# Attention, routed experts and a feed-forward in one launch: the turn tables move from VectorE to GpSimd, and the rank products go one chunk later

## Chip, cores and metric

One core of a Trainium2 chip runs the whole program in one launch. The metric is the device time in microseconds, the median of several runs. The profiled execution is one more, with its own time. Engines are named as in the profile: PE (TensorE), DVE (VectorE), ACT (ScalarE), POOL (GpSimd), SP (SyncE, which only issues DMAs here).

## What is computed

A linear attention with a decaying state over 768 steps (batch 4, 8 heads of 48), its rows as 3072 tokens of 384 into a top-1 mixture of 8 experts, and a dense feed-forward with an ELU:

```python
for t in range(S):
    kt, vt, rt = (k[:, :, t], v[:, :, t], r[:, :, t])
    cur = np.einsum('bhd,bhe->bhde', u[None] * kt, vt)
    y[:, :, t] = np.einsum('bhd,bhde->bhe', rt, state + cur)
    state = w[None, :, :, None] * state + np.einsum('bhd,bhe->bhde', kt, vt)
...
expert_idx = np.argmax(x @ w_gate, axis=1)
for e in range(E):
    mask = expert_idx == e
    out[mask] = gate_w[mask, None] * (np.maximum(x[mask] @ w1[e], 0.0) @ w2[e])
...
g = np.where(h > 0.0, h, np.exp(np.minimum(h, 0.0)) - 1.0)   # h = x @ w_in
return g @ w_out
```

## The kernel before

Every engine has its own program, written out by hand; within one the order is that of the code, and between them only semaphores order the work. There are three stages.

**Attention** (to about 156 us). The 768 steps are cut into 6 chunks of 128, for 4 batches b: 24 chunks n = 6b + c. Per chunk PE makes the scores (`heads`, line 1348), the state products (`new_state`, line 1369, which need `v_in`), what the old state gives (`old`, 1382, which needs `xT` of the chunk before), the rows and gate logits of the chunk before (`rows_logits`, 1407), the own term (`own_sum`, 1359) and the masked part (`inside`, 1393). DVE scales the next chunk's r and k, masks the scores, renews the state, reduces the logits (`lgt`), and makes `own` and `xT`. POOL scales the keys (`keys`, tile `kn_s`), makes `rk` and scatters finished rows, tagged with token and gate, into `x_sorted` in HBM, expert by expert. SP loads r, k, kn, vT and v of the chunks to come into pairs of buffers: in its round n `load_rk(n + 1)`, which waits for `scaled` and `rk_done`, then `load_v(n)`, then a piece of expert weights.

Once per batch, at c = 0, DVE chooses experts (`choose`, which ends with the one-hot `hot`), PE turns `hot` into ranks within each expert (`ranks`, lines 1421 to 1424, into PSUM), and DVE makes row numbers and gates of them (`place`, from `rank_e` to the reciprocal). The last batch is placed in two groups, the first four chunks at c = LAST = 4, the other two after the end.

While the attention runs, the weights of two experts are loaded in 24 pieces and split into a high and a low part (`expert_highs` on ACT, `first_experts` on POOL). Pieces 0 to 11 are of expert 0. Pieces 12 to 23 are of the fullest other expert after two batches: DVE's `pick_first` finds it at chunk FIRST = 12, from the counts that `ranks` leaves in PSUM, and signals `first_ok`; SP waits for that in its round 14 and reads the expert into a register. In which order the experts take their turns, and where their tiles begin, follows in five steps on DVE, `turns_a` to `turns_e`, in chunks 13 to 17. `split_now` says which pieces are split in chunk n: before chunk 12 piece n, from 14 on piece n - 2, and pieces 22 and 23 after the last chunk.

**Expert tiles** (156 to 462 us). 31 tiles of 128 rows. Per tile: gather `xg` (ACT issues it), transpose (`x_pose`, line 1457), split into hi and lo, up product (`first_up` or `up`), relu, transpose `hs` (`h_pose`, 1487), split into `hThi` (ACT) and `hTlo` (DVE), down product. Tile 0 is of the picked expert and needs no table. For the others DVE computes tables from the final counts: `fill_row` (where each expert's rows end), `past`, `tile_row`, `tile_turn`, `end_i`, `tile_start`. SP fills the rows behind each expert's last with zeros, eight DMAs in the order of turns: two as soon as `fill_row` is there (`fill_in`), the others when all scatters have landed (`fill2_in`, and `fills_in` for the last five), and then loads the weights of turn 2. ACT may gather tile i only when the fills that it could touch are in; for i = 3 it waits for all of them.

**Feed-forward** (462 to 880 us), with which the change has nothing to do.

## Time and profile before

| | us |
|---|---|
| runs | 893.85, 893.48, 890.81 (median 893.48) |
| the profiled execution | 888.82 |
| its span, first to last instruction | 887.1 |
| PE busy in it | 851.8 (96%) |
| DVE, ACT, POOL busy | 411.5, 246.4, 399.2 |
| mean granted TensorE clock | 0.992 |

The span is that of one execution, 1.7 us shorter than its time. Busy times overlap; an engine that is idle may be waiting or have nothing to do. In the timeline a row is a start, a duration, an engine, a line of the kernel and what it writes and reads; a bracket at its end is how long the engine sat idle before it and what released it. SPq and ACTq are the DMA issues of an engine, whose durations are those of the issue, not of the transfer. DVE was busy for 11.2 of the 12 us from 82 to 94.

### The profile page before, as it was taken

The numbers are of one execution on the slowest core, as the hardware profiler recorded it, in microseconds if no ns is written. First come the engines' busy times: TensorE is split into PE (matmuls) and PEld (weight loads), VectorE is DVE, ScalarE is ACT, GpSimd is POOL, SyncE is SP. The second block draws the span as 40 slices with busy tenths as digits, with TensorE's granted clock in tenths as the row PEclk, the third lists the DMA queues.
The fourth block names the chain that finished last, engine by engine and source line by source line (L and its number), as shares of the span: only waits on it lengthen the run. The fifth ranks groups of instructions, "written<-read, shape, count | busy, mean of one in ns | idle before, by whom it ended". The sixth has DMA issues, their size and how long they took to land.

```text
span 887.1 us, 16841 instructions
## 1 busy us (share of the span) xinstructions
PE 851.8 (96%) x5278; PEld 770.8 (87%) x5278; DVE 411.5 (46%) x842; ACT 246.4 (28%) x514; POOL 399.2 (45%) x286
## 2 busy tenths in 40 slices
PE   5999989879999999999999999999999999999996
PEld 5888988669999999999988899988999989998895
DVE  7888997625444444434335553332333232332221
ACT  3333232212222222222223343222332223232221
POOL 7677677207575734437102223423423422433424
PEclk9999999989999999999999999999999999999998
DMA  7877986353445335164121000100100100000000
GB/s 181 235 230 235 238 237 192 126 178 117 149 145 177 118 117 176 48 228 147 37 63 45 19 19 10 45 19 1 54 18 1 44 27 0 35 0 0 36 1 36
DMA packets 48991, 83.96 MB, mean 95 GB/s; under 512 B 6816, under 2 KB 27040, under 8 KB 48544
## 3 DMA queue, kind: packets, MB, share of 16 engines
q1 hardware_dynamic: 35808, 60.59, 22.8%
q10 hardware_dynamic: 10048, 13.04, 4.6%
q0 software_dynamic: 3072, 9.46, 2.8%
q8 instruction: 42, 0.69, 0.3%
q14 instruction: 21, 0.17, 0.1%
HBM read 65.92 MB, written 17.15 MB: 94 GB/s over the span
## 4 chain that ended last, share of the span: by engine, by line
PE 78%; issue 12%; DVE 4%; POOL 3%; DMA 2%; SPq 1%; POOLq 0%; ACT 0%; ACTq 0%; DVEq 0%
PE bank L1462 10%; PE bank L1464 10%; PE bank L1463 9%; PE bank L1574 6%; PE bank L1576 6%; PE bank L1575 6%; PE bank L1593 5%; PE bank L1595 5%; PE bank L1594 5%; PE bank L1487 3%; PE bank L1393 2%; PE bank L1348 2%; PE bank L1382 2%; PE bank L1407 2%; POOL glo L669 2%
## 5 line engine op out<-in xcount | busy, mean ns | idle before, releaser
L669 POOL TENSOR_TENSOR glo<-gf,ghi 128x512 fp32r<-128x512 f32 x96 | 123.8, 1290 | 303.9 <-ACT ghi L1291 303.9
L1072 DVE TENSOR_SCALAR he<-he 128x512 f32<-128x512 f32 x96 | 41.0, 427 | 241.0 <-ACT he L1309 240.9
L1309 ACT ACTIVATE he<-bank 128x512 f32<-128x512 f32 x96 | 57.5, 599 | 253.5 <-PE bank L1576 253.5
L1593 PE MATMUL bank<-wout_hi,ghi 128*128 128x384 f32 x376 | 126.1, 335 | 0.3 <-issue 0.3
L1595 PE MATMUL bank<-wout_hi,glo 128*128 128x384 f32 x376 | 126.1, 335 | 0.0
L1594 PE MATMUL bank<-wout_lo,ghi 128*128 128x384 f32 x376 | 126.0, 335 | 0.0
L1574 PE MATMUL bank<-x2hi,win_hi 128*128 128x512 f32 x288 | 115.7, 402 | 0.0
L1576 PE MATMUL bank<-x2hi,win_lo 128*128 128x512 f32 x288 | 114.1, 396 | 0.0
L1575 PE MATMUL bank<-x2lo,win_hi 128*128 128x512 f32 x288 | 113.5, 394 | 0.0
L1462 PE MATMUL bank<-w_sb,hThi 128*128 x248 | 87.5, 353 | 4.8 <-DVE hTlo L938 2.9
L1464 PE MATMUL bank<-w_sb,hTlo 128*128 x248 | 84.6, 341 | 0.0
L1463 PE MATMUL bank<-w_sb,hThi 128*128 x248 | 84.6, 341 | 0.0
L1593 PEld LDWEIGHTS bank<-wout_hi,ghi 128*128 128x128 f32 x376 | 70.7, 188 | 4.7 <-issue 0.7
L1594 PEld LDWEIGHTS bank<-wout_lo,ghi 128*128 128x128 f32 x376 | 70.6, 188 | 4.5
L1462 PE MATMUL bank<-w_sb,xhi 128*128 x180 | 73.1, 406 | 1.0 <-issue 1.0
L1595 PEld LDWEIGHTS bank<-wout_hi,glo 128*128 128x128 f32 x376 | 70.6, 188 | 0.0
L1464 PE MATMUL bank<-w_sb,xlo 128*128 x180 | 70.6, 392 | 0.0
L1463 PE MATMUL bank<-w_sb,xhi 128*128 x180 | 70.1, 389 | 0.0
L1076 DVE SCALAR_TENSOR_TENSOR gf<-bank,he 128x512 f32<-128x512 f32 x96 | 66.4, 692 | 3.7
L1576 PEld LDWEIGHTS bank<-x2hi,win_lo 128*128 128x128 f32 x288 | 54.1, 188 | 13.3
L1219 ACT ACTIVATE hThi<-bank 128x512 fp32r<-128x512 f32 x62 | 33.7, 596 | 104.3 <-PE bank L1487 104.3
L1574 PEld LDWEIGHTS bank<-x2hi,win_hi 128*128 128x128 f32 x288 | 54.2, 188 | 9.1 <-issue 0.4
(214 smaller groups left out, 1502.5 us busy)
## 6 DMA issues: line engine op xcount, KB each, us to landing
w_raw_up<-w SPq DMA_DIRECT2D x12, 768.0 KB, 6.2
w_raw_down<-w SPq DMA_DIRECT2D x12, 768.0 KB, 7.0
w_raw<-w SPq DMA_DIRECT2D x24, 256.0 KB, 4.1
y_rows<-ye ACTq DMA_DIRECT2D x31, 192.5 KB, 2.5
xg<-x_sorted ACTq DMA_DIRECT2D x30, 193.0 KB, 2.8
k_in<-kT SPq DMA_DIRECT2D x48, 96.0 KB, 3.4
r_in<-rT SPq DMA_DIRECT2D x48, 96.0 KB, 3.7
kn_in<-kn SPq DMA_DIRECT2D x24, 192.0 KB, 3.8
```

The source lines that it names most:

```text
L669: pool.tensor_tensor(glo[f % GS][:, :], gf[f % 2][:, :], ghi[f % GS][:, :].bitcast(F32), ALU.subtract).then_inc(s.g_lo, 1)
L1076: dve.scalar_tensor_tensor(gf[f % 2][:, :], bank[1 + f % 2][:, :], 0.0, he[f % 2][:, :], ALU.max, ALU.add).then_inc(s.g_done, 1)
L1309: act.activation(he[f % 2][:, :], bank[1 + f % 2][:, :], ACT.Exp).then_inc(s.exp_done, 1)
L1462: pe.matmul(out, hi, w, start=first, stop=False)
L1463: pe.matmul(out, hi, w_low, start=False, stop=False)
L1464: return pe.matmul(out, lo, w, start=False, stop=last)
L1574: pe.matmul(bank[1 + f % 2][:, :], win_hi[:, k, cols], x2hi[par][:, k, :], start=(k == 0), stop=False)
L1575: pe.matmul(bank[1 + f % 2][:, :], win_hi[:, k, cols], x2lo[par][:, k, :], start=False, stop=False)
L1576: last = pe.matmul(bank[1 + f % 2][:, :], win_lo[:, k, cols], x2hi[par][:, k, :], start=False, stop=(k == KD - 1))
L1593: pe.matmul(to, ghi[f % GS][:, rows], wout_hi[:, f, :], start=(f == 0), stop=False)
L1594: pe.matmul(to, ghi[f % GS][:, rows], wout_lo[:, f, :], start=False, stop=False)
L1595: last = pe.matmul(to, glo[f % GS][:, rows], wout_hi[:, f, :], start=False, stop=(f == KF2 - 1))
```

## The change

It touches the order of the work in the attention, who makes the turn tables, and the passage to the expert tiles.

1. `ranks` and `place` move from chunk c = 0 to c = 1 (and from LAST to LAST + 1): PE multiplies behind the next chunk's scores, DVE places between that chunk's `own` and `xT`. `pick_first` moves from chunk 12 to 13. SP's wait for `first_ok` stays in round 14.
2. `turns_a` to `turns_e` are taken off DVE. POOL makes the same tables in one go in round 15 (`turn_tables`, 29 instructions, six waits on its own semaphore), after its split and before its scatter, plus two helper values, `row_step` and `other_row`.
3. Splits run one chunk closer: pieces 12 and 13 in chunk 14, then n - 1, and 22 and 23 in chunk 23, on ACT, POOL and in SP's rounds (where the order of the loads stays as it was).
4. SP reads all eight turns into registers ahead of the fills; the fourth fill signals `fill3_in` on its own.
5. DVE makes `next_row`, the row of tile 1, early from the first expert's count (four instructions more), and puts `gid` and `hTlo` of tile 0 ahead of `past`. ACT gathers tile 1 by `next_row`, and gathers tile 3 before the relu of tile 1.

```diff
         def split_now(n):
-            return [n] if n < FIRST else ([n - 2] if n >= FIRST + 2 else [])
+            if n < FIRST:
+                return [n]
+            if n < FIRST + 2:
+                return []
+            return {FIRST + 2: [n - 2, n - 1], NT - 1: [n - 1, n]}.get(n, [n - 1])
@@ SP @@
+            sp.wait_ge(s.turns_ok, 1)
+            turns = [sp.value_load(turn_expert[0:1, turn:turn + 1], min_val=0, max_val=E - 1) for turn in range(E)]
             def fill(turn, done):
-                e = sp.value_load(turn_expert[0:1, turn:turn + 1], min_val=0, max_val=E - 1)
+                e = turns[turn]
...
             fill(2, s.fill2_in)
-            for turn in range(3, E):
+            fill(3, s.fill3_in)
+            for turn in range(4, E):
                 fill(turn, s.fills_in)
@@ POOL, batch @@
+                    if n == FIRST + 3:
+                        turn_tables()
...
+            def turn_tables():
+                pool.wait_ge(s.first_ok, 1)
+                pool.tensor_scalar(pull[:, :], most[:, :], float(P), None, ALU.is_lt)
+                pool.tensor_scalar(is_first[:, :], iota_e[:, :], first[:, 0:1], None, ALU.is_equal)
...
+                pool.tensor_tensor(ahead[:, :, :], turn_of[:, :].unsqueeze(1).to_broadcast([P, E, E]),
+                                   turn_of[:, :].unsqueeze(2).to_broadcast([P, E, E]), ALU.subtract)
...
+                pool.tensor_copy(turn_expert[:, :], self_1[:, :])
+                pool.tensor_tensor(row_step[:, :], row_step[:, :], first_mul[:, :], ALU.add).then_inc(s.turns_ok, 1)
@@ DVE, batch @@
-                    if c == 0 and not fresh:
+                    if c == 1 and not fresh:
                         place(0, NC, b - 1, b - 1, b > 2)
-                    if last and c == LAST:
+                    if last and c == LAST + 1:
                         place(0, LAST, b, b, True)
                     x_columns(n, c % 2, fresh and c < 2)
-                    if n == FIRST:
+                    if n == FIRST + 1:
                         pick_first()
-                    if FIRST < n <= FIRST + 5:
-                        (turns_a, turns_b, turns_c, turns_d, turns_e)[n - FIRST - 1]()
@@ DVE, routing @@
+            rlink(dve.tensor_tensor(from_first[:, :], n_e[:, :], is_first[:, :], ALU.mult))
+            rlink(dve.tensor_reduce(n_first[:, :], from_first[:, :], AX.X, ALU.add))
+            rlink(dve.tensor_scalar(n_first[:, :], n_first[:, :], float(P), row_step[:, 0:1], ALU.is_gt, ALU.mult))
+            dve.tensor_scalar(next_row[:, :], n_first[:, :], other_row[:, 0:1], None, ALU.add).then_inc(s.next_row_ok, 1)
...
+            gate_and_id(0, 0, True)
+            v_hT(0, 0, True)
             rlink(dve.tensor_tensor(past[:, :, :], index[:, :].unsqueeze(2).to_broadcast([P, NI, E]),
...
-            gate_and_id(0, 0, True)
-            v_hT(0, 0, True)
@@ ACT @@
+            act.wait_ge(s.next_row_ok, 1)
+            act.wait_ge(s.fill_in, 32)
+            load_x(1, 1, next_row)
             act.wait_ge(s.rows_ok, 1)
-            act.wait_ge(s.fill_in, 32)
-            load_x(1, 1)
             act.wait_ge(s.fill2_in, 16)
             next_x(2, 0)
             a_x(1, xhi[1], True)
+            act.wait_ge(s.fill3_in, 16)
+            next_x(3, 1)
             a_relu(1, 1, True)
             a_x(2, xhi[0], False)
             a_hT(1, 1, True)
-            act.wait_ge(s.fills_in, 16 * (E - 3))
-            next_x(3, 1)
@@ PE, batch @@
+                    if c == 1 and b:
+                        ranks(NC, b - 1)
+                    if last and c == LAST + 1:
+                        ranks(LAST, b)
                     if c < NC - 1:
                         new_state(b, c, c % 2)
                     old(b, c, c % 2).then_inc(s.old_done, 1)
                     rows_logits(n - 1, (c - 1) % 2, fresh and c == 1)
                     own_sum(n, c % 2, False)
-                    if c == 0:
-                        ranks(NC, b - 1)
-                    if last and c == LAST:
-                        ranks(LAST, b)
```

On PE, in chunk 12, before: from `own_sum` (`rk`) to the scores of chunk 13; `hot` is the one-hot, `allb` and `ltri` are constant matrices.

```order
L1359 MATMUL bank<-rk_97,spread_u 128x128 x4
L1421 MATMUL bank<-hot_116,allb 128x8 x7
L1422 MATMUL bank<-hot_116,ltri 128x48
L1424 MATMUL bank<-hot_116,allb 128x48
L1424 MATMUL bank<-hot_116,allb 128x40
L1424 MATMUL bank<-hot_116,allb 128x32
L1424 MATMUL bank<-hot_116,allb 128x24
L1424 MATMUL bank<-hot_116,allb 128x16
L1424 MATMUL bank<-hot_116,allb 128x8
L1393 MATMUL bank<-am_101,v_in_91 48x128 x8
L1348 MATMUL bank<-r_s_94,k_s_96 128x128 x8
```

The same place after; the scores of chunk 13 are the row with `r_s_95`, and line numbers are those of the changed kernel:

```order
L1381 MATMUL bank<-rk_98,spread_u 128x128 x4
L1415 MATMUL bank<-am_102,v_in_92 48x128 x8
L1370 MATMUL bank<-r_s_95,k_s_97 128x128 x8
L1443 MATMUL bank<-hot_117,allb 128x8 x7
L1444 MATMUL bank<-hot_117,ltri 128x48
L1446 MATMUL bank<-hot_117,allb 128x48
L1446 MATMUL bank<-hot_117,allb 128x40
L1446 MATMUL bank<-hot_117,allb 128x32
L1446 MATMUL bank<-hot_117,allb 128x24
L1446 MATMUL bank<-hot_117,allb 128x16
L1446 MATMUL bank<-hot_117,allb 128x8
L1391 MATMUL bank<-v_in_93,kn_s_101 112x96 x4
```

The products stood ahead of `inside` (`am`) of chunk 12; now `inside` and the next scores go first and the products stand between these and the state products.

On DVE, from `own` of chunk 12 on, before:

```order
L750 TENSOR_TENSOR own_103<-vT_in_87,bank 128x512
L808 TENSOR_TENSOR rank_e<-bank,hot_116 128x48
L810 TENSOR_REDUCE rank<-rank_e 128x6
L816 SCALAR_TENSOR_TENSOR pos_i_58<-bank,rank 128x6
L818 TENSOR_REDUCE l_sum<-l_exp 128x6
L820 RECIPROCAL xt<-l_sum 128x6
L770 TENSOR_TENSOR xT_105<-bank,own_103 128x512
L832 TENSOR_REDUCE most<-bank 128x1
L833 SCALAR_TENSOR_TENSOR from_first<-bank,most,rev_in 128x7
L834 TENSOR_REDUCE rev_best<-from_first 128x1
L835 TENSOR_SCALAR first<-rev_best 128x1
L836 CAST first_expert<-first 128x1
```

After, `own` and `xT` of chunk 12 follow each other, and this stands in chunk 13, from its `own` on:

```order
L805 TENSOR_TENSOR own_105<-vT_in_89,bank 128x512
L863 TENSOR_TENSOR rank_e<-bank,hot_117 128x48
L865 TENSOR_REDUCE rank<-rank_e 128x6
L871 SCALAR_TENSOR_TENSOR pos_i_58<-bank,rank 128x6
L873 TENSOR_REDUCE l_sum<-l_exp 128x6
L875 RECIPROCAL xt<-l_sum 128x6
L825 TENSOR_TENSOR xT_107<-bank,own_105 128x512
L887 TENSOR_REDUCE most<-bank 128x1
L888 SCALAR_TENSOR_TENSOR from_first<-bank,most,rev_in 128x7
L889 TENSOR_REDUCE rev_best<-from_first 128x1
L890 TENSOR_SCALAR first<-rev_best 128x1
L891 CAST first_expert<-first 128x1
```

`place` (`rank_e` to `xt<-l_sum`) and `pick_first` (`most` to `first_expert`) are one whole chunk of DVE's work further back; what stood behind them, the scaling of the next chunk, now runs ahead of them.

On ACT, around the relu of tile 1 (`hs`), before; `xg_182` is the gather of tile 2, `xg_183` that of tile 3:

```order
L1199 DMA xg_182<-x_sorted 128x386
L1145 ACTIVATE xhi_127<-bank 128x384
L1212 ACTIVATE hs_131<-bank 128x512
L1145 ACTIVATE xhi_126<-bank 128x384
L1219 ACTIVATE hThi_133<-bank 128x512 x2
L1198 TENSOR_LOAD tile_row
L1198 ISA x2
L1199 ISA
L1199 DMA xg_183<-x_sorted 128x386
```

After, with `xg_189` for tile 2 and `xg_190` for tile 3:

```order
L1219 DMA xg_189<-x_sorted 128x386
L1167 ACTIVATE xhi_128<-bank 128x384
L1218 TENSOR_LOAD tile_row
L1218 ISA x2
L1219 ISA
L1219 DMA xg_190<-x_sorted 128x386
L1232 ACTIVATE hs_132<-bank 128x512
L1167 ACTIVATE xhi_127<-bank 128x384
L1239 ACTIVATE hThi_134<-bank 128x512 x2
```

The gather of tile 3 stood behind the relu, the split of tile 2 and `hThi` of tile 1; now it stands directly behind the split of tile 1's rows (`xhi`).

## Rows read from the trace of the kernel before

**Rows 1.** The page, part 1: busy us (share of the span) and instructions of each engine.
```profile
PE 851.8 (96%) x5278; PEld 770.8 (87%) x5278; DVE 411.5 (46%) x842; ACT 246.4 (28%) x514; POOL 399.2 (45%) x286
```

**Rows 2.** Timeline, PE: start us, us, engine line op out<-in xcount; chunks 13 and 15.
```profile
88.01 1.16 PE L1348 MATMUL bank<-r_s,k_s 48*128 48x128 f32 x16
...
100.63 1.02 PE L1369 MATMUL bank<-v_in,kn_s 128*112 128x96 f32 x8
```

**Rows 3.** Timeline, PE: rank products of chunks 6, 12, 18; in brackets the wait before.
```profile
51.79 0.18 PE L1422 MATMUL bank<-hot,ltri 128*128 128x48 bf16 x1 [0.86 <-DVE hot L798]
...
86.58 0.32 PE L1421 MATMUL bank<-hot,allb 128*128 128x8 bf16 x7 [0.67 <-DVE hot L798]
...
123.80 0.18 PE L1422 MATMUL bank<-hot,ltri 128*128 128x48 bf16 x1 [1.27 <-DVE hot L798]
```

**Rows 4.** Timeline, PE: waits for VectorE in chunks 15 and 17.
```profile
104.81 1.08 PE L1393 MATMUL bank<-am,v_in 128*48 128x128 f32 x16 [0.45 <-DVE am L743]
...
113.06 1.13 PE L1382 MATMUL bank<-r_s,state 128*128 128x128 f32 x8 [0.29 <-DVE xT L770]
...
116.70 1.08 PE L1393 MATMUL bank<-am,v_in 128*48 128x128 f32 x16 [0.72 <-DVE am L743]
```

**Rows 5.** Timeline, DVE and SyncE's queue: the chosen expert, and v of chunk 15.
```profile
89.57 0.15 DVE L836 CAST first_expert<-first 128x1 int32<-128x1 f32 x1
...
95.02 0.35 SPq L431 DMA_DIRECT2D v_in<-vn  x1
```

**Rows 6.** DMA issues of 95.0 to 95.3 us: KB each, us from issue to landing.
```profile
v_in<-vn SPq DMA_DIRECT2D x1, 192.0 KB, 4.4
```

**Rows 7.** Instructions of tile v_in: its DMAs' landing times.
```profile
DMA to landing us min/median/max: 2.4/3.7/5.2
```

**Rows 8.** Timeline, DVE: place of chunk 12, and own of chunk 13.
```profile
87.23 0.20 DVE L808 TENSOR_TENSOR rank_e<-bank,hot 128x48 f32<-128x48 f32 x1
...
88.13 0.69 DVE L770 TENSOR_TENSOR xT<-bank,own 128x512 f32<-128x512 f32 x1
...
93.08 0.69 DVE L750 TENSOR_TENSOR own<-vT_in,bank 128x512 f32<-128x512 f32 x1
```

**Rows 9.** Timeline, POOL and DVE: small and large instructions.
```profile
43.48 0.14 POOL L544 IOTA iota_e<- 128x8 f32 x1
...
100.76 1.28 POOL L583 TENSOR_TENSOR w_sb<-w_raw,w_sb 128x512 fp32r<-128x512 f32 x1
...
100.94 1.19 DVE L849 TENSOR_TENSOR ahead<-turn_of 128x64 f32<-128x64 f32 x1
...
203.58 6.82 POOL L576 TENSOR_TENSOR w_sb<-w_raw_up,w_sb 128x3072 fp32r<-128x3072 f32 x1 [0.19 <-POOL w_sb L573]
```

**Rows 10.** Instructions of tile kn_in: ns min/median/max, first and last start.
```profile
L564 POOL TENSOR_TENSOR kn_s<-kn_in,pw_kn x24: 991/1001/1020, 13.2 to 142.0; 128x384 f32<-128x384 f32 x24
```

**Rows 11.** Timeline, DVE and SyncE's queue, after the attention.
```profile
159.70 0.95 DVE L972 TENSOR_TENSOR fill_row<-n_e,first_row 128x8 int32<-128x8 f32 x1
...
162.13 14.12 SPq L463 DMA_DIRECT2D x_sorted<-zeros  x8
```

**Rows 12.** Timeline, PE: the first product of first_down.
```profile
166.06 0.68 PE L1462 MATMUL bank<-w_sb,hThi 128*128 x1 [2.88 <-DVE hTlo L938]
```

**Rows 13.** Windows: us, busy us by engine, PEclk (1.00 is 2.4 GHz), DMA share, GB/s.
```profile
166.00:168.00 2.00, 1.95 (x6) 1.95 (x7) 1.72 (x8) 0.00 (x0) 0.00 (x0) 0.50 0.28 97
...
189.00:191.00 2.00, 2.00 (x6) 2.00 (x7) 0.37 (x1) 0.00 (x0) 0.00 (x0) 0.50 0.31 112
```

**Rows 14.** Timeline, PE: x_pose of i=3, then x_pose and down around i=4.
```profile
187.35 0.90 PE L1457 MATMUL bank<-ident,xg 128*128 128x128 f32 x3 [3.54 <-DMA xg<-x_sorted]
...
200.13 0.49 PE L1457 MATMUL bank<-ident,xg 128*128 128x128 f32 x3
...
200.37 0.42 PE L1462 MATMUL bank<-w_sb,hThi 128*128 x1
```

**Rows 15.** The chain that ended last: start us, us, what.
```profile
179.56 7.75 DMA xg<-x_sorted
```

83 lines of the change are left out of this document (45 added, 38 removed).

## Prediction

> **What bounds the kernel now.** I read the page first: PE is busy for 96% of the span [rows 1], so a change of other engines' work pays only where PE waits. Then I looked for PE's waits in the timeline. From 195 us to the end the trace shows PE almost without one (the loop over sorted tiles has none), so the change can act only in the attention chunks (23 to 156 us) and in the passage to the expert tiles (156 to 193 us). In the attention two undisturbed chunks and one set of scores take 12.62 us (88.01 to 100.63) [rows 2], that is 5.76 a chunk. PE waits there for two reasons: at the rank products of chunks 6, 12 and 18 (and 22), for `hot` (0.86, 0.67, 1.27) [rows 3], and behind the turn steps that VectorE (DVE) fits into chunks 13 to 17 (0.45 in chunk 15, 0.29 and 0.72 in chunk 17) [rows 4]. In the passage it waits 2.88 us for `hTlo` and 3.54 us for the gathered tile `xg` of i=3, and after both gaps the granted clock is half, 1.2 GHz [rows 12 to 14].
>
> **Part 1, ranks one chunk later.** Behind the scores of the next chunk, `hot` is long there: in chunk 12 the products began at 86.58, the scores of 13 stand at 88.01 and last 1.1. The products themselves (0.25 to 0.42 us) stay. Gain 0.86+0.67+1.27 = 2.8 us. The wait of chunk 22 is given back: `place` for it now stands in chunk 23 between `own` and `xT`, and the last logits wait for that `xT`; `place` takes 1.3 us there, about what the waits around it took. Zero.
> `place` in the other batches is 0.90 us from `rank_e` to `xT` (87.23 to 88.13) [rows 8]. In chunks 7 and 13 it fits: `xT` then starts 6.8 to 7.0 us after the chunk's scores, and the next chunk's state product needs it at 8.0. In chunk 19, where it waits for slots (1.6 us in the profile), `xT` is 0.3 us late. Cost 0.3.
>
> **Part 2, turn steps off DVE.** Gain 0.45+0.29+0.72 = 1.5 us in chunks 15 and 17.
>
> **Part 3, the new lateness of `first_expert`.** SyncE's queue (SP) waits for `first_ok` in its round 14, and that wait is not moved, but `pick_first` is, from chunk 12 to chunk 13, behind that chunk's `own`, the `place` and `xT`. Queued behind the wait are the weight pieces 12 and 13, then k, r, kn of chunk 16, and v of chunk 15. Let T be the start of chunk 13's scores (88.01). Now: `first_expert` is done at 89.72, T+1.71; v of chunk 15 goes out at 95.02, 5.30 us after it, without a pause between its DMAs, and lands 4.4 us later at 99.4 [rows 5, 6]; PE needs it at 100.63 [rows 2]. Slack 1.2 us. Then: `own` of chunk 13 starts at T+5.07 (93.08) [rows 8] plus 0.42 for the rank products that now precede it, T+5.49; 0.59 to `place`, 0.90 to `xT`, and 1.59 from the start of `xT` to the end of `first_expert` (88.13 to 89.72): T+8.57. v goes out at T+13.87 and lands at T+18.27. PE is ready for it at 12.62 + 0.42 = T+13.04. **PE waits 5.2 us.** The bounds: landing in 3.7 us (median of v) 4.5; with 5.2 (longest) 6.0 [rows 7]. After gaps of 2.9 and 3.5 us the clock was half for 3 to 4 us of work [rows 13]; in the second the first twelve products took 4.0 us, where twelve at full clock take 2.1. So 1.8 us more. Cost 7.0 us, none of it in the trace of before. ScalarE and GpSimd (POOL) wait for the late pieces 12 and 13 too, but until T+14.9 and T+16.3 only, under PE's wait.
>
> **Part 4, turn tables on POOL.** 29 small instructions and six waits for its own results, in round 15, ahead of a scatter and of keys and `rk` of chunk 17, on which SP's loads for chunk 19 wait, and behind those v of chunk 18. The trace has no such instruction. From below: IOTA on 128x8 takes 0.14, the seven of them one every 0.1 us [rows 9], giving 3.5 us with the waits (0.19 each, as between POOL's own splits (203.58) [rows 9]). From above: two points of its elementwise form, 1.0 us for 384 columns and 1.28 for 512 [rows 9, 10], leave some 0.2 at nothing, giving 7.5. I take 5.3, between them, since pipelined starts are nearer to the IOTA row. Starting at T+21.6 (piece 14 lands at T+19.5, its split ends then), `rk` of chunk 17 is done 3.4 us after the tables, T+30.3, v of chunk 18 goes out 3.3 us later and lands at T+37.5; PE wants it at T+36.5. Cost 1.0 (0 to 3.2); no cost up to 4.3 us of tables. In chunk 19 POOL must wait for the later `place` before its two scatters, which sets v of chunk 22 back: 0.6 (0 to 0.9).
> A row on how the two engines meet: DVE's `ahead`, 64 columns, took 1.19 us and ended at 102.13, where POOL's subtraction ended at 102.04 [rows 9]; `fill_row` took 0.95 [rows 11] with POOL's last splits running until 160.63. The Trainium skill ("SBUF — State Buffer", section "Who interferes with whom") has it that a VectorE instruction with two SBUF inputs waits for a GpSimd instruction that reads SBUF, and that whichever came first holds the shared port. By that rule `fill_row` shrinks to 0.2, since those splits are now earlier; if the 0.95 were its own, the gain of part 5 would be 0.5 us less. The big VectorE instructions of a chunk read PSUM, so by the rule they don't hold the tables up.
>
> **Part 5, the passage.** (a) `hTlo` of tile 0 stands behind the tile tables; now ahead of `past`. `hThi` is ready at 163.3 and 163.9, four added instructions (0.9 us) take the place of the 0.75 that `fill_row` loses, so the two `hTlo` (0.64 each) end at 164.65 rather than 165.79: first_down starts 1.15 us earlier. PE's gap becomes 1.75 us (from 163.17). The clock fell within gaps of 2.9 and 3.5 us and not in one of 1.27 [rows 3, 12 to 14]; I take that it stays up, 1.4 us more. (b) `xg` of i=3 is issued at 179.56, after 3 MB of weights from 177.04 on, and lands 7.75 us later; PE is ready at 183.66 and begins at 187.35 [rows 14, 15]. Now it is issued ahead of relu(1), when `gid` of tile 1 and the fourth fill are there, at about 171, and has 10 us. Its wait goes, and with it the half clock: the twelve products after it ended at 192.98; at the pace of i=4 (200.13, 200.37) [rows 14] (0.24 and 12 x 0.175 us) they end at 186.0. Gain 7.0. (c) Fills go from 1.8 us apart (eight in 14.12) [rows 11] to some 1.1, one register load less. The second fill then lands at about 164.1, the last scatter at 164.4, `xg` of i=1 goes out at 165.1 and lands 2.7 later at 167.8; the earlier first_down reaches its transposition after 18 products, at 168.0. Just in time. It also starts the weights at 171.3; POOL needs these at 200 only. Nothing by itself. What is late next: PE itself. Sum 1.15+1.4+7.0 = 9.5 us.
>
> **Sum**, against the profiled execution (888.82 us, span 887.1): -2.8 -1.5 +7.0 +0.3 +1.0 +0.6 -9.5 = -4.9 us, 883.9. The median of the runs shown is 4.66 above that execution; the same 0.55% off 893.48 gives **888.6**.
>
> **Rivals.**
> *The loads come in time.* SP has been still for 8 us, so transfers could land faster, in 2.4 us as the fastest v did, with POOL light: waits of 3 us without the clock falling long, or less. Or the wait is hidden in a way I don't see. Without part 3: -4.9 -7.0 = -11.9 us, 881.6. For it: DMA was busy all along before this burst and is idle now. Against: the issue times alone (T+13.87) are past PE's T+13.03.
> *POOL and SP don't catch up.* Tables at 7.5 us, the v of chunk 18 3 us late and the clock falling again, first_down's clock gain missing: -4.9 +2.2 +1.8 +1.4 = +0.5, 894. For it: POOL then has splits, tables and scatters in a row, and the loads wait for `rk`.
> *Slower.* POOL's tables alone, if its small instructions take 0.45 us each: 13 us of tables put the v of chunk 18 out by 9 us, and a second half-clock stretch: -4.9 +8 +1.8 = +4.9, 898.4. It decides from 13 us of tables on. Against: the IOTA of 8 columns takes 0.14 [rows 9].
> *It doesn't do what it says.* `xg` of i=3 could still be late, if the fourth fill or `gid` of tile 1 came after the weights and it landed no sooner; it would need 11 us against the 7.75 seen. Then -4.9 +7 = +2.1, 895.6. I give it 3 of 100.
>
> **How the numbers follow.** The forecast as worked (-2.5 to -7.5) 50%; in time 20%; not catching up 20%; slower 5%; doesn't do what it says 3%; else 2%. A measurement tells about 0.5%, 4.5 us, from no change; the forecast lies just beyond, so I count 35 of its 50 as faster and 15 as same. Faster 0.35+0.20+0.02, same 0.15+0.17+0.02, slower the rest. Range: from the case without the wait, 881, to the one without catching up, 894, with 2 in 10 left out.
>
> **What would show it.** PE's `v_in` product of chunk 15 with a DMA wait of 4 to 6 us and half clock after it, SP's `v_in` issue some 14 us after chunk 13's scores; no wait at the rank products; tables on POOL in 4 to 7 us; `hTlo` of tile 0 ahead of `past`, PE's gap 1.8 us at full clock; no wait for `xg` at i=3. I am wrong if chunk 15 runs through, if the tables take over 10 us, or if something after 195 us moves.

## The result, and the profile after

The changed kernel took 897.96 us (median of 12 runs, 895.65 to 902.39), the kernel before 891.38 us on the same chip (12 runs, 888.98 to 893.85): **ratio 1.0079, 95% interval 1.006 to 1.0097**, slower by some 7 us where 4.9 less were forecast. The forecast's range ended at 894. The profiled execution took 900.95 us with a span of 899.2; a second profile of the same kernel (a0 below) is of an execution of 893.28 us with a span of 891.6. The median of 897.96 lies between the two, so both are read below.

The page of after, part 1; [rows 1] answer to it. PE has 4.3 us more busy time for the same number of instructions, at a mean granted clock of 0.985 against 0.992:

```profile
span 899.2 us, 16856 instructions
PE 856.1 (95%) x5278; PEld 775.5 (86%) x5278; DVE 407.5 (45%) x827; ACT 247.6 (28%) x514; POOL 405.0 (45%) x315
```

The timeline of after, PE, where it waits in the attention, and the rank products of chunk 13. Columns as in the rows of before:

```profile
83.26 1.71 PE L1391 MATMUL bank<-v_in,kn_s 128*112 128x96 f32 x8 [1.87 <-DMA v_in<-vn]
90.85 0.18 PE L1444 MATMUL bank<-hot,ltri 128*128 128x48 bf16 x1
107.62 1.81 PE L1391 MATMUL bank<-v_in,kn_s 128*112 128x96 f32 x8 [4.97 <-DMA v_in<-vn]
130.87 1.81 PE L1391 MATMUL bank<-v_in,kn_s 128*112 128x96 f32 x8 [4.88 <-DMA v_in<-vn]
158.09 1.47 PE L1391 MATMUL bank<-v_in,kn_s 128*112 128x96 f32 x8 [1.85 <-DMA v_in<-vn]
```

The rank products wait for nothing now (against 0.67 to 1.27 us in [rows 3]). In their place PE waits for v in chunks 12, 15, 18 and 22 (and 0.65 us in chunk 10). The windows of after at chunk 15 show the clock behind such a wait (the number after POOL's):

```profile
core 0: us, PE busy (x) PEld busy (x) DVE busy (x) ACT busy (x) POOL busy (x), PEclk, DMA share, GB/s
107.60:109.60 2.00, 1.98 (x10) 1.99 (x11) 0.75 (x2) 0.63 (x1) 1.69 (x3) 0.50 1.08 234
109.60:111.60 2.00, 2.00 (x15) 2.00 (x15) 0.52 (x2) 0.00 (x0) 2.00 (x4) 0.72 1.05 312
111.60:113.60 2.00, 2.00 (x27) 1.84 (x26) 1.07 (x3) 1.45 (x5) 1.77 (x8) 1.00 1.05 290
```

A chunk lasts from its scores to the next chunk's. Worked out from the starts of the scores in both timelines:

| chunk | before, us | after, us | more |
|---|---|---|---|
| 12 | 81.08 to 88.01 | 80.23 to 89.56 | 2.40 |
| 15 | 99.54 to 105.83 | 101.48 to 113.74 | 5.97 |
| 18 | 117.71 to 125.06 | 124.83 to 137.31 | 5.13 |
| 22 | 142.35 to 148.97 | 155.08 to 164.38 | 2.68 |
| start of first_up | 156.67 | 172.81 | 16.14 |

The four chunks make 16.18 us, as much as the whole attention lost; what the other chunks gained (the rank products of chunk 6, the turn steps of chunk 17) and lost (chunk 10) cancels. The passage gives some of it back.

Why v was late is in POOL's and SP's queues. POOL in after, three places: the first scatter of a batch, in POOL's round 13, the turn tables (first and last of 29 instructions), and what follows them; then SP's loads behind `rk`:

```profile
97.44 1.01 POOL L610 DMA_INDIRECT x_sorted<-xt,pos_i  x1 [7.36 <-issue]
...
110.78 0.25 POOL L647 TENSOR_SCALAR pull<-most 128x1 f32<-128x1 f32 x1
...
117.84 0.19 POOL L676 TENSOR_TENSOR row_step<-row_step,first_mul 128x1 f32<-128x1 f32 x1
118.76 1.11 POOL L610 DMA_INDIRECT x_sorted<-xt,pos_i  x1 [0.73 <-PE bank L1381]
119.90 1.01 POOL L577 TENSOR_TENSOR kn_s<-kn_in,pw_kn 128x384 f32<-128x384 f32 x1
120.86 1.28 POOL L571 TENSOR_TENSOR rk<-r_in,k_in 128x512 f32<-128x512 f32 x1
```

```profile
122.17 0.33 SPq L427 DMA_DIRECT2D k_in<-kT  x1
...
125.41 0.39 SPq L445 DMA_DIRECT2D v_in<-vn  x1
```

POOL stands 7.36 us at the scatter (1.86 in the kernel before, its row at 89.22), until `place`, now one chunk further back in DVE's order, is done (its last instruction ends at 96.42). The same scatter stands 5.04 us in round 7 and 6.14 in round 19. The keys and `rk` of the chunks to come are queued behind it, SP waits for `rk` with its next load of k, and v is queued behind that. The tables take 7.25 us; k goes out as soon as `rk` ends (122.14), v 3.24 us later, and it lands 5.4 us after that (the prediction had counted 3.9), when PE has stood 4.88 us.

The passage in after: relu of tile 0 on ACT, then PE at first_down, at up of tile 2 and at the gathered tile i=3, for which it doesn't wait:

```profile
180.60 0.60 ACT L1248 ACTIVATE hs<-bank 128x512 f32<-128x512 f32 x1 [7.07 <-remote]
```

```profile
184.19 0.68 PE L1484 MATMUL bank<-w_sb,hThi 128*128 x1 [1.79 <-DVE hTlo L956]
198.48 0.50 PE L1484 MATMUL bank<-w_sb,xhi 128*128 x1 [0.77 <-issue]
202.72 0.49 PE L1479 MATMUL bank<-ident,xg 128*128 128x128 f32 x3
```

The gap before first_down is 1.79 us (2.88 in [rows 12]). From the start of `up` of tile 2 to the end of the span it takes 899.2 - 198.48 = 700.7 us, where before took 887.1 - 179.45 = 707.65: 6.9 us less, since x of tile 3 is there. ACT began the relu at 180.60, though the last product of first_up ended at 177.48: 3.1 us that nothing in the trace accounts for.

### The profile page after: what moved, and what is told of

The parts are those of the page before. It is cut to its first block, busy times and chain, and to the rows that moved or that the text cites. A ratio compares the mean times of both kernels' runs of the same rounds, so it can differ in the third digit from the quotient of the medians.

```text
span 899.2 us, 16856 instructions
## 1 busy us (share of the span) xinstructions
PE 856.1 (95%) x5278; PEld 775.5 (86%) x5278; DVE 407.5 (45%) x827; ACT 247.6 (28%) x514; POOL 405.0 (45%) x315
## 4 chain that ended last, share of the span: by engine, by line
PE 75%; issue 12%; POOL 5%; DMA 4%; SPq 2%; DVE 1%; another core or an unknown queue 1%; ACT 0%; POOLq 0%; DVEq 0%; ACTq 0%
PE bank L1484 10%; PE bank L1486 9%; PE bank L1485 9%; PE bank L1596 5%; PE bank L1597 5%; PE bank L1598 5%; PE bank L1615 5%; PE bank L1616 5%; PE bank L1617 5%; PE bank L1509 3%; DMA v_in<-vn 3%; PE bank L1404 2%; POOL glo L724 2%; PE bank L1391 2%; PE bank L1429 2%
## 5 line engine op out<-in xcount | busy, mean ns | idle before, releaser
L1598 PEld LDWEIGHTS bank<-x2hi,win_lo 128*128 128x128 f32 x288 | 54.1, 188 | 13.1
```

Of the source, the lines that this page charges most:

```text
L1598: last = pe.matmul(bank[1 + f % 2][:, :], win_lo[:, k, cols], x2hi[par][:, k, :], start=False, stop=(k == KD - 1))
```

## Experiments

Each part alone, from the kernel before; then parts mended, from the kernel after. Ratios are to the kernel before on the same chip, and 0.001 is 0.9 us.

| kernel | ratio | 95% interval |
|---|---|---|
| the change | 1.0079 | 1.006 to 1.0097 |
| a0, the change again | 1.009 | 1.0058 to 1.0121 |
| p1, ranks alone | 1.0137 | 1.0101 to 1.0173 |
| p2, passage alone | 0.9935 | 0.9911 to 0.9959 |
| p3, tables alone | 1.0029 | 1.0014 to 1.0045 |
| p4, splits alone | 0.9985 | 0.9972 to 0.9998 |
| x1, pieces later | 1.0026 | 1.0009 to 1.0043 |
| x2, scatters later | 1.0028 | 1.0011 to 1.0044 |
| x3, tables in pieces | 1.001 | 0.9992 to 1.0027 |
| x4, all three | 0.9932 | 0.9907 to 0.9957 |
| x5, x4 and v first | 0.9915 | 0.9882 to 0.9948 |
| x8, x1 + x2, tables on DVE | 0.9979 | 0.996 to 0.9999 |
| x9, change, PE kept busy | 1.0058 | 1.0041 to 1.0075 |
| x10, passage + tables in pieces | 0.9916 | 0.9883 to 0.9949 |
| x12, x4, PE busy in passage | 0.9938 | 0.9915 to 0.9961 |
| x13, ranks alone, mended | 0.9979 | 0.9964 to 0.9995 |
| x15, x10, PE busy in passage | 0.9908 | 0.988 to 0.9936 |

The parts alone add up: +12.2 +2.6 -5.8 -1.3 = +7.7 us (ratios by 890 us), and the change measured +7.0 and +8.0. That is in part chance: p1 holds two long waits that the change doesn't have, and p2 a cost of 1.75 us of its own (both below).

### p1: the ranks alone

```diff
@@ DVE: place, pick_first; PE: ranks, as in the change @@
-                    if FIRST < n <= FIRST + 5:
-                        (turns_a, turns_b, turns_c, turns_d, turns_e)[n - FIRST - 1]()
+                    if FIRST + 1 < n <= FIRST + 6:
+                        (turns_a, turns_b, turns_c, turns_d, turns_e)[n - FIRST - 2]()
```

> The kernel before, with only the rank products on PE, place, pick_first and the turn steps on DVE one chunk later (POOL's scatters, the turn tables on DVE, the splits and the passage as before). Theory (moving place one chunk later holds POOL at its first scatter of a batch and SP at first_ok, and the late v that follows costs a gap and a stretch of half clock each time): the three waits for ranks of PE (2.8 us) go; waits for v come in chunks 10 and 12 (0.6 and 1.4 to 1.9 us), 15 (5 us) and 22 (1 to 2 us), with 1.7 us of half clock behind each of the longer three: -2.8 + 0.6 + 3.4 + 6.8 + 3.2 = +11, ratio to the kernel before 1.012. Rival (the terms of the prediction: only chunk 15 is late): -2.8 + 0.3 + 7.0 = +4.5, ratio 1.005.

The loss was as large as the theory of late loads said, and some 7 us above the prediction's terms for this part (-2.8 +0.3 +7.0 +0.6 = +5.1). PE's waits in p1, and POOL at its first scatter in chunk 7:

```profile
103.33 1.81 PE L1369 MATMUL bank<-v_in,kn_s 128*112 128x96 f32 x8 [4.67 <-DMA v_in<-vn]
123.13 1.08 PE L1393 MATMUL bank<-am,v_in 128*48 128x128 f32 x16 [2.73 <-DVE am L743]
154.84 1.53 PE L1369 MATMUL bank<-v_in,kn_s 128*112 128x96 f32 x8 [2.15 <-DMA v_in<-vn]
181.18 0.68 PE L1462 MATMUL bank<-w_sb,hThi 128*128 x1 [5.12 <-DVE hTlo L938]
```

```profile
58.36 1.17 POOL L597 DMA_INDIRECT x_sorted<-xt,pos_i  x1 [5.38 <-issue]
```

Chunks 15 and 22 wait as named. Chunk 12 waited less than expected (0.60), and two waits came that neither side had named: 2.73 us for `am` of DVE, and 5.12 us for `hTlo`. Ahead of each, a small DVE instruction had run long beside POOL (a turn step 1.71 us from 118.82, `more` 3.41 us from 172.68); x8 and x13 take that up. So the agreement of 12.2 us with the 11 expected is in part luck: chunk 12 cost less, and these two cost what nobody had counted.

### x1, x2, x3, x4: one mend each, and all

x1 moves SP's wait for `first_ok`, and all pieces, one round on. x2 moves the scatters one round on. x3 cuts the tables into seven pieces behind each of POOL's six waits for its own results (`plink`), one piece in each of rounds 15 to 21.

```diff
@@ x1 @@
-            if n < FIRST + 2:
+            if n < FIRST + 3:
                 return []
-            return {FIRST + 2: [n - 2, n - 1], NT - 1: [n - 1, n]}.get(n, [n - 1])
+            return {FIRST + 3: [n - 3, n - 2], NT - 2: [n - 2, n - 1], NT - 1: [n - 1, n]}.get(n, [n - 2])
...
-                if n == FIRST + 2:
+                if n == FIRST + 3:
                     sp.wait_ge(s.first_ok, 1)
@@ x2 (the last batch likewise: two in rounds c = 2, 3, 4) @@
-                        if c and not fresh:
-                            scatter_x(b - 1, c - 1, b - 1)
+                        if c > 1 and not fresh:
+                            scatter_x(b - 1, c - 2, b - 1)
                         elif b > 1:
-                            scatter_x(b - 2, NC - 1, b - 2)
+                            scatter_x(b - 2, NC - 2 + c, b - 2)
@@ x3 @@
-                    if n == FIRST + 3:
-                        turn_tables()
+                    if FIRST + 3 <= n < FIRST + 10:
+                        turn_tables(n - FIRST - 3)
```

> The changed kernel, but SP waits for first_ok (and loads the first piece of the chosen expert, and the splits on POOL and ACT follow) one round later, at n = FIRST + 3. Theory (each late load has a cause of its own, and the one of chunk 15 is SP's wait for first_ok with the v of that chunk queued behind it): the 4.97 us wait of PE in chunk 15 and the 1.8 us of half clock behind it go, the waits in chunks 12, 18 and 22 stay; 898.0 - 6.8 = about 891. Rival (SP is late anyway, since its loads of k and r wait for a late POOL): the wait only moves to chunk 16 or stays, 896 to 898.

> The changed kernel, but POOL issues each scatter of a batch one round later, so that it no longer stands at its first scatter until the later place on DVE is done. Theory (POOL held at the scatter is late with the products, SP is held by rk_done and loads v late): the waits of PE in chunks 10 and 12 (0.65 and 1.87 us) and 22 (1.85 us), each with about 1.7 us of half clock for the longer two, go; 898.0 - 7.8 = about 890; the waits in chunks 15 and 18 stay at about 5 us each. Rival (SP's own slow issues make v late): chunks 12 and 22 wait as before, 897 to 898.

> The changed kernel, but POOL makes the turn tables in seven pieces, one in each of the rounds 15 to 21, instead of in one row of 29 instructions in round 15. Theory (the 7.25 us row on POOL delays the products of the next chunk, so k, r and then v are late): the 4.88 us wait in chunk 18 and 1.8 us of half clock go, chunks 12, 15 and 22 stay; 898.0 - 6.7 = about 891. Rival (chunk 18 is late since POOL never caught up after the late pieces of weights of chunk 15; the tables only add to it): the wait in chunk 18 shrinks by less than half, 895 to 897.

> The changed kernel with all three edits: pieces of weights one round later, scatters one round later, turn tables in seven pieces. Theory (the causes are separate and add up): no wait of PE for v over 1 us, clock never at half before the passage; 898.0 - 6.8 - 7.8 - 6.7 = 877 if all of it adds, 880 if the chunks left are as long as the 5.76 us of an undisturbed one and the passage is as it was. Rival (POOL is simply full in the last batch: splits, tables, scatters and products together take longer than the chunks, and the wait moves to chunks 20 to 23): 886 to 892.

Against the change (1.0079), x1 gained 4.7 us, x2 4.5, x3 6.1, and all three 13.1. PE's waits in each: x1, which lost chunk 15's wait and got a wait for `rk` in chunk 17:

```profile
82.98 1.02 PE L1391 MATMUL bank<-v_in,kn_s 128*112 128x96 f32 x8 [1.55 <-DMA v_in<-vn]
117.85 1.71 PE L1381 MATMUL bank<-rk,spread_u 128*128 128x128 f32 x8 [1.83 <-POOL rk L571]
125.74 1.81 PE L1391 MATMUL bank<-v_in,kn_s 128*112 128x96 f32 x8 [3.10 <-DMA v_in<-vn]
154.62 1.02 PE L1391 MATMUL bank<-v_in,kn_s 128*112 128x96 f32 x8 [2.37 <-DMA v_in<-vn]
```

x2, which has only chunks 15 and 18 left:

```profile
103.59 1.81 PE L1391 MATMUL bank<-v_in,kn_s 128*112 128x96 f32 x8 [5.31 <-DMA v_in<-vn]
126.89 1.81 PE L1391 MATMUL bank<-v_in,kn_s 128*112 128x96 f32 x8 [5.11 <-DMA v_in<-vn]
```

x3, chunks 12, 15 and 21 (not shown are 0.56 us in chunk 10, 0.28 in 19 and 0.88 in 22); chunk 18 ran through:

```profile
82.32 1.25 PE L1398 MATMUL bank<-v_in,kn_s 128*112 128x96 f32 x8 [1.36 <-DMA v_in<-vn]
106.41 1.81 PE L1398 MATMUL bank<-v_in,kn_s 128*112 128x96 f32 x8 [4.72 <-DMA v_in<-vn]
143.74 1.02 PE L1398 MATMUL bank<-v_in,kn_s 128*112 128x96 f32 x8 [0.72 <-DMA v_in<-vn]
```

x4, all waits for v that are left:

```profile
115.68 1.02 PE L1398 MATMUL bank<-v_in,kn_s 128*112 128x96 f32 x8 [0.80 <-DMA v_in<-vn]
122.90 1.02 PE L1398 MATMUL bank<-v_in,kn_s 128*112 128x96 f32 x8 [1.12 <-DMA v_in<-vn]
135.59 1.02 PE L1398 MATMUL bank<-v_in,kn_s 128*112 128x96 f32 x8 [0.79 <-DMA v_in<-vn]
```

So each late v has its own cause, as the theory had it: `first_ok` for chunk 15, the held scatter for 10, 12 and 22, the row of tables for 18. It isn't quite as clean in the last batch, where x3 has less of a wait in chunk 22 too, and x1 less in 18 (3.10 us, but a0, the change again, has 2.82 there). Against the terms of their expectations (6.8, 7.8, 6.7) they fell short by 2.1, 3.3 and 0.6 us. These had been made from the first profile of the change, the longer one, and x1 turned part of its gain into a wait for `rk`. x4 missed its 877 to 880: three waits of about 1 us stay in the last batch, where POOL has splits, scatters and tables in every round, and the clock fell in first_up, behind a gap of 1.29 us for `xT`.

### p3: the tables alone

```diff
@@ POOL: turn_tables in round 15, as in the change @@
@@ DVE: turns_a to turns_e left out @@
```

> The kernel before, with only the turn tables moved from DVE to POOL (in round 15, in one row of 29 instructions of 7.25 us). Theory (POOL has room only as long as no scatter and no piece holds it): the DVE waits of 1.5 us go, one wait of PE for rk or v of 1 to 3 us comes in chunks 17 or 18 with up to 1.7 us of half clock: +1 to +3, ratio 1.001 to 1.004. Rival (as early as first_ok is in the kernel before, the row is caught up behind the slack of the loads and POOL costs nothing): -1.5, ratio 0.998. Rival 2 (the row alone makes the whole wait of chunk 18): 4.9 + 1.8 - 1.5 = +5, ratio 1.006.

```profile
119.60 1.80 PE L1384 MATMUL bank<-v_in,kn_s 128*112 128x96 f32 x8 [3.75 <-DMA v_in<-vn]
```

The tables alone make a wait of 3.75 us in chunk 18, where the two profiles of the change have 4.88 and 2.82. The time, +2.6 us, is that of the first theory, since DVE's own waits went with its steps.

### p2: the passage alone

```diff
@@ SP, ACT, DVE behind the attention: as in the change @@
@@ DVE, turns_e: row_step and other_row @@
+                tlink(dve.tensor_scalar(other_row[:, :], first_base[:, :], float(-E * REG), pull[:, 0:1], ALU.add, ALU.mult))
+                dve.tensor_scalar(first_mul[:, :], pull[:, :], -float(P), float(P), ALU.mult, ALU.add)
...
```

> The kernel before, with only the passage of the change: SP reads the turns before the fills and signals the fill of turn 3 by itself, x of the first two tiles is loaded from next_row and behind fill3_in, and DVE makes the low half of hT ahead of the routing tables; row_step and other_row are made by DVE beside its turn steps. Theory (as predicted): -1.15 for hTlo, -1.4 where the clock stays up, -7.0 for x of i = 3: -8.2 to -9.5, ratio 0.990. Rival (x of i = 3 lands late in the absence of a longer attention as well, or the work behind only waits for the weights): -1 to -3, ratio 0.997 to 0.999.

It gained 5.8 us. Behind `up` of tile 2 the span has 882.0 - 181.48 = 700.5 us left, 7.1 less than before: x of tile 3 is worth what was forecast. first_up began 1.75 us later than before, since the five instructions added to DVE lengthen the waits there, as at chunk 18's rank products (1.27 in [rows 3]). The change has these on POOL, so this cost is p2's own:

```profile
125.33 0.18 PE L1445 MATMUL bank<-hot,ltri 128*128 128x48 bf16 x1 [2.00 <-DVE hot L810]
```

And the earlier `hTlo` brought nothing in this profile. first_down in p2:

```profile
166.78 0.68 PE L1485 MATMUL bank<-w_sb,hThi 128*128 x1 [1.87 <-DVE hTlo L955]
```

```profile
core 0: us, PE busy (x) PEld busy (x) DVE busy (x) ACT busy (x) POOL busy (x), PEclk, DMA share, GB/s
168.00:170.00 2.00, 2.00 (x8) 2.00 (x7) 1.84 (x7) 0.00 (x0) 0.00 (x0) 0.50 0.43 121
170.00:172.00 2.00, 2.00 (x8) 2.00 (x7) 0.33 (x2) 0.00 (x0) 0.00 (x0) 0.50 0.76 272
172.00:174.00 2.00, 2.00 (x12) 1.86 (x11) 0.21 (x1) 0.49 (x1) 0.00 (x0) 0.81 0.57 134
```

The gap is 1.0 us shorter, but 18 of the 24 products run at half clock, where it was 9 in the kernel before, and first_down takes 1.3 us longer by that. In other profiles the earlier `hTlo` did pay: from the start of first_up to `up` of tile 2 it takes 22.78 us in the kernel before, 23.06 in p2, but 21.87 in a0, 21.67 in x2, 21.85 in x3 and 21.86 in x9. a0 and x2 have no half clock there and the other two have some 3 us of it, and they end almost alike: in a0 PE waits for the gathered tile 1 (0.69 us) and for `xlo` (0.99) instead. So the earlier `hTlo` was worth 0.9 to 1.1 us, and a clock that stays up 0.2 at most.

### x9, x12 and x15: PE kept busy while it waits

These add matmuls whose results are overwritten, so that PE doesn't stand still; nothing that it waits for comes earlier.

```diff
@@ x9, new_state: 2, 5, 5, 2 times in chunks 12, 15, 18, 22 @@
+                for _ in range({12: 2, 15: 5, 18: 5, 22: 2}.get(n, 0)):
+                    for g in range(G):
+                        kn2 = kn_s[slot][:, 2 * g:2 * g + 2, :].rearrange("p h d -> p (h d)")
+                        pe.matmul(ps_m[0:64 + DH, g, :, :].rearrange("p a d -> p (a d)"), kn2[:, 0:64 + DH], kn2[:, 0:2 * DH], start=True, stop=True)
                 pe.wait_ge(s.v_in_s[slot], 16 * (n // 2) + 16)
@@ x12 and x15, first_down @@
+                for _ in range(8):
+                    pe.matmul(bank[5][:, 0:D], xhi_first[:, 0, :], w_sb[:, bass.ds(sl, 1), 0, 0, 0:D].rearrange("p o f -> p (o f)"), start=True, stop=True)
                 pe.wait_ge(s.hTlo_done, 2)
```

> The changed kernel, but PE multiplies kn_s by itself into ps_m (which new_state overwrites) while it waits for v: 16 matmuls in chunks 12 and 22 and 40 in chunks 15 and 18, about as long as its waits there. v comes no earlier; what goes is only that PE stands still. Theory (each of the four waits costs a stretch of half clock of 1.7 to 1.8 us beside itself): granted clock 1.0 throughout chunks 12 to 22, 4 x 1.75 = 7 us less than the changed kernel, ratio to the kernel before 1.000. Rival (the chunk behind a late v is long for another reason, such as DVE and ACT catching up): no change against the changed kernel, ratio 1.006 to 1.010.

> The kernel with the three edits (ratio 0.993), and PE makes 8 matmuls of 128x384 into bank 5 (overwritten by first_down) between h_pose and its wait for hTlo. Theory (the 1.8 us gap, after the 0.7 us one, is what brings the clock down in first_down): first_down runs at full clock, 18 matmuls x 0.15 us = 2.6 us less, ratio 0.990. Rival (the gap before h_pose has brought the clock down already, or the extra matmuls delay first_down by as much as they save): ratio 0.993 or more.

> The kernel before with the passage and the tables on POOL in seven pieces (ratio 0.9916), and PE makes 8 matmuls of 128x384 into bank 5 between h_pose and its wait for hTlo. Theory (first_down then runs at full clock, and first_up runs at full clock already in this kernel): 1.6 to 2.6 us less, ratio 0.989 to 0.990. Rival (what first_down gains, up of the next tile loses waiting for its xlo): ratio 0.991 to 0.992.

x9 at chunk 15: the state products behind the added ones, the next scores, and the stretch that answers to 107.6 to 109.6 of the change:

```profile
105.89 1.02 PE L1395 MATMUL bank<-v_in,kn_s 128*112 128x96 f32 x8 [0.35 <-DMA v_in<-vn]
110.57 1.16 PE L1370 MATMUL bank<-r_s,k_s 48*128 48x128 f32 x16
```

```profile
107.00:109.00 2.00, 2.00 (x20) 2.00 (x19) 0.90 (x3) 0.61 (x2) 1.72 (x3) 1.00 1.03 267
```

The clock is 1.00 from chunk 12 to 22. What the half clock costs is read from the start of the state products, when v is there in each, to the next chunk's scores:

| chunk | the change, us | a0, us | x9, us |
|---|---|---|---|
| 12 | 6.30 | 4.67 | 4.67 |
| 15 | 6.12 | 7.32 | 4.68 |
| 18 | 6.44 | 6.30 | 4.67 |
| 22 | 6.29 | 6.31 | 4.67 |

a0's chunk 12 waited 0.73 us and kept its clock. In its chunk 15 the half clock lasts for 5.6 us behind the wait (to 111.0), in the other stretches for 3.1 to 3.7. So the half clock is a price of its own: 1.4 to 1.8 us a stretch, 2.6 for the long one, and 6.5 us in the four chunks of the change's profile, near the 7 expected. The times of the runs don't show so much: x9 is 1.9 us below the change's 1.0079 and 2.8 below a0, and the intervals overlap, so that gain isn't clear of noise. In a0 v came earlier in chunks 12 and 18 (0.73 and 2.82 us of waiting), where x9 multiplies for 1.8 and 4.1 us and would hold PE up; whether that is why the times gained less is not shown.

In x12 and x15 first_down ran at full clock from its first product to its last. In x15 PE then stood 1.33 us for the gathered tile 1, and from first_up to `up` of tile 2 it took 22.27 us, in x10 22.24: the clock gained there is lost to the next transfer, as the rival had it. Neither gained time: 0.9938 against x4's 0.9932, and 0.9908 against x10's 0.9916.

### x13, x8, p4: what is left of the ranks, the tables' engine, the splits

x13 is p1 with the scatters and the pieces one round later, x8 the change with both and the tables in five steps of DVE.

```diff
@@ x13, on p1; scatters as in x2 @@
-            return [n] if n < FIRST else ([n - 2] if n >= FIRST + 2 else [])
+            return [n] if n < FIRST else ([n - 3] if n >= FIRST + 3 else [])
@@ p4, on the kernel before: split_now as in the change @@
```

> The kernel before with the ranks, place and pick_first one chunk later (ratio 1.0137 alone), and also POOL's scatters and the pieces of the chosen expert (SP's wait for first_ok, the splits on POOL and ACT) one round later. Theory (the loss of that part is POOL standing at its first scatter and SP at first_ok, and nothing in the rank products themselves): no wait for v over 1 us, ratio 0.999 to 1.002. Rival (half of the loss is in DVE's turn steps and the later places, which stand between DVE's own steps): ratio 1.006 or more.

> The changed kernel with pieces and scatters one round later and the turn tables made by DVE in five steps in rounds 14 to 18 (five instructions more for row_step and other_row) instead of POOL. It differs from the kernel with the three edits (ratio 0.993) by the engine of the tables. Theory (steps of 8 elements on DVE stand for 1.0 to 1.7 us where POOL works beside them, and PE then waits for am or xT): +2 us, ratio 0.995 to 0.997. Rival (POOL full in the last batch is worth as much as DVE's steps): ratio 0.993.

> The kernel before, with only the rule on the pieces changed: POOL and ACT split each piece of the chosen expert one round earlier (in SP's order), two in round 14 and two in round 23, none behind the last chunk. Theory (a side matter): ratio 0.999 to 1.001. Rival (POOL stands in round 14 until the first piece of the chosen expert has landed and ACT has rounded it, and the products behind it are late): +2 to +4 us, ratio 1.002 to 1.005.

x13 settles p1: with POOL no longer held and `first_ok` out of the way, the part goes from 1.0137 to 0.9979, and no wait for v is left. Its first_up begins at 154.09, 2.6 us before that of the kernel before, near the 2.8 us of rank waits that the prediction counted. It lost part of this again in the passage, where DVE and POOL in x13 show:

```profile
157.75 3.85 DVE L973 TENSOR_TENSOR fill_row<-n_e,first_row 128x8 int32<-128x8 f32 x1
```

```profile
157.85 3.73 POOL L584 TENSOR_TENSOR w_sb<-w_raw,w_sb 128x512 fp32r<-128x512 f32 x3
```

An instruction on 8 columns lasted 3.85 us, until POOL's third split in a row was over (161.58). In the kernel before it was 0.95 [rows 11]; in the change, whose splits end before it, 0.17 (at 176.55). x8 shows the same in the attention, DVE then POOL:

```profile
104.26 1.36 DVE L857 SCALAR_TENSOR_TENSOR from_first<-is_first,first,from_first 128x8 f32<-128x8 f32 x1
105.66 0.17 DVE L858 SCALAR_TENSOR_TENSOR turn_of<-iota_e,from_first 128x8 f32<-128x8 f32 x1
105.86 1.30 DVE L859 TENSOR_TENSOR ahead<-turn_of 128x64 f32<-128x64 f32 x1
```

```profile
104.30 1.28 POOL L570 TENSOR_TENSOR rk<-r_in,k_in 128x512 f32<-128x512 f32 x1
105.81 1.27 POOL L595 TENSOR_TENSOR w_sb<-w_raw,w_sb 128x512 fp32r<-128x512 f32 x1 [0.22 <-ACT w_sb L1140]
```

Two steps end with the POOL instruction beside them, within 0.1 us, and the one between two of POOL's takes 0.17. The Trainium skill ("SBUF — State Buffer", section "Who interferes with whom") gives the cause as one pair of ports that a VectorE instruction with two inputs in SBUF shares with GpSimd. The rows agree. So the turn steps are dear on DVE and cheap on POOL if cut up: x8 is 0.0047 (4 us) above x4.

p4 stayed just below 1 (its interval ends at 0.9998): the earlier splits cost nothing and bring about 1 us.

### a0, x5 and x10

```diff
@@ x5, on x4: SP loads v(n) ahead of k, r, kn of n + 1 @@
-                if n < NT - 1:
-                    load_rk(n + 1, (n + 1) % 2, n == 0)
                 if n:
                     load_v(n, n % 2, n < 2)
+                if n < NT - 1:
+                    load_rk(n + 1, (n + 1) % 2, n == 0)
@@ x10, on the kernel before: the passage as in p2, tables on POOL as in x3 @@
```

> The changed kernel once more, for a second profile. Theory (the 3.1 us that ACT stood between the end of first_up and hs in the first profile belong to that one execution: no instruction that it waits for ends then): hs starts within 0.1 us of the end of first_up, the gap of PE before h_pose is 0.69 us, the waits for v in chunks 12, 15, 18 and 22 are those of the first profile within 0.6 us; ratio 1.008 to the kernel before. Rival (the order of ACT's stream in this kernel makes it): the gap is 3 to 4 us again.

> The kernel with all three edits (pieces and scatters one round later, tables in seven pieces; ratio 0.993 to the kernel before), and SP loads v of chunk n before k, r and kn of chunk n + 1. Theory (v is late because it is queued behind k and r, whose load waits for POOL's products): v comes by 2 to 3 us earlier, the three waits of PE that are left in the last batch (0.80, 1.12 and 0.79 us) go: ratio 0.990. Rival (SP then stands at y_psum of the chunk before, and k and r come late instead, so that heads waits for the scaling on DVE in chunk after chunk): slower than the kernel with the three edits, ratio 0.995 or more.

> The kernel before with the passage of the change and the turn tables on POOL in seven pieces in rounds 15 to 21; rank products, place and pick_first stay where they were. Theory (moving the ranks is worth its 2.8 us of PE waits only if the late place costs nothing; the passage is worth 6.9 and turn steps off DVE 1.5 to 3): 890 - 6.9 - 1.5 = 881.5 to 882, ratio 0.991, within 1 us of the kernel with the three edits. Rival (without the later ranks the attention keeps its waits and with them stretches of half clock): ratio 0.994 to 0.996, slower than the kernel with the three edits.

In a0 the relu starts as first_up ends, the gap of PE before `h_pose` is 0.69 us:

```profile
173.89 0.60 ACT L1248 ACTIVATE hs<-bank 128x512 f32<-128x512 f32 x1 [3.95 <-PE bank L1486]
```

So ACT's 3.1 us belong to that one execution (no other profile shows them), and what held ACT stays open. The waits for v come again at 0.73, 4.80, 2.82 and 1.79 us. Chunk 15's and 22's are steady, chunk 12's and 18's moved by 1.1 and 2.1 us, more than the 0.6 expected, and chunk 10's grew from 0.65 to 1.44. first_up begins at 169.20 here, 12.5 us later than in the kernel before, against 16.1 in the first profile: the loss of the attention varies by 3.6 us between two executions.

x5 is 0.9915 against x4's 0.9932, and the intervals overlap: no difference shown. No wait for v is left in it; PE waits for `kn_s` of POOL instead, up to 1.79 us. So with v loaded first, it is POOL's products that PE waits for in the last batch.

x10 is as fast as x4 with nothing moved but the passage and the tables. Its rank products wait as before (0.87, 0.67, 0.67 and 0.58 us), and three of its chunks wait for v (0.50, 0.36 and 1.33 us), as three do in x4. x4, x5, x10 and x15 all take 881 to 882 us, against 888 to 891 of the kernel before, and their intervals overlap. **All four beat both kernels, and x10 and x15 get there without the part that moves the ranks.**

## The prediction, point by point

- **Part 1 is the step that failed.** The waits for the ranks went, and without them, the scatters and pieces mended, the attention is 2.6 us shorter (x13). But the step "in chunks 7 and 13 it fits" looked at `xT` and at PE alone. For these chunks it did not ask who else waits for `place`: POOL's first scatter of the batch, with keys and `rk` queued behind it, which SP's next load waits for, with v behind that. The prediction did name that wait in part 4, but for chunk 19 alone, at 0.6 us for chunk 22; there it measured 1.85 us of wait and 1.6 of half clock. The trace of before had the row, POOL 1.86 us idle at the scatter of round 13; in the change it is 7.36. That is chunks 10, 12 and 22, longer by 0.72, 2.40 and 2.68 us in the first profile, and 4.5 us by x2. (p1's two other long waits, for `am` and for `hTlo`, aren't in the change.)
- **Chunk 15 (part 3)** was right: v goes out 14.6 us after chunk 13's scores (104.14 against 89.56; forecast 13.87), PE waits 4.97 us (5.2), the chunk is 5.97 us longer (7.0). x1, where the wait is gone, and x2, where it stays at 5.31, show it as `first_ok`'s alone.
- **Part 4 mis-sized one term.** 29 instructions take 7.25 us, not 5.3; 7.5 was the upper bound. From the IOTA row the forecast took one instruction every 0.1 us, and POOL's small ones came every 0.14 to 0.41. The model behind it, no cost up to 4.3 us of tables, gives 3.0 us of wait for 7.25, and p3 has 3.75; in the change v also landed 1.5 us later than assumed. The half clock behind the wait was not in the sum. The gain from DVE (part 2) is real, and larger than the 1.5 counted by the three gaps: 4 us between x8 and x4, with the five instructions for `row_step` and `other_row` among them.
- **The clock** was counted as falling behind gaps of 2.9 us and more, and not behind 1.27. It fell behind waits of 1.87 and 1.85 us too (windows at 0.60 and 0.62 there), so chunks 12 and 22 paid twice, 1.6 us each beside the wait. The price of 1.8 us for a stretch was about right (1.4 to 1.8, and 2.6 once).
- **Part 5, x of tile 3:** 7.0 forecast, 6.9 and 7.1 measured. **hTlo:** 1.15 forecast, 1.0 to 1.1 off the gap, and 0.9 to 1.1 kept in a0, x2, x3 and x9. **"I take that it stays up, 1.4 us more"** failed twice over: in eleven profiles with this passage and no matmuls added to it, the clock stayed up in first_down in two and fell in nine, eight of them behind gaps like those of the two; and where it did stay up, the next tile was late instead. Passage -9.5 forecast, -5.8 measured in p2, which paid 1.75 for its own steps on DVE and had 18 products at half clock.
- **fill_row** shrank from 0.95 to 0.17 (0.2 forecast).
- **The sum:** -4.9 forecast, +7.0 measured. By part, with the 0.6 of chunk 19 counted where it belongs: ranks and `first_ok` +5.1 against +12.2, tables -0.5 (with part 2) against +2.6, passage -9.5 against -5.8, splits 0 against -1.3. The rival "POOL and SP don't catch up" named the loads waiting for `rk`, but gave the tables as the reason. The slower rival (5%) named 898.4 us, next to the 897.96 measured, and that is luck: it had tables and a late v in chunk 18 right, but wanted 13 us of tables, where 7.25 and the held scatters, which it left out, were enough.

## What to carry to other kernels

When a step moves later, list everyone who waits for it, not only the engine for which it is moved. Follow each in-order queue behind the wait to what it feeds: here `place` to POOL's scatter, to `rk`, to SP's load of k, to v, to PE. Before a row of small instructions goes onto a queue that feeds loads, cut it into pieces no longer than the slack of the loads: the same 29 instructions cost 6 us less in seven pieces than in one row (x3), and chunk 18 ran through. Price a gap of PE with the half clock behind it (1.4 to 1.8 us here), and count no gain from a clock that only may stay up, nor from one whose work then waits for the next tile.
